# Windowed attention and two expert layers on one core: Q, K and V laid out ahead of the launch, K's key ranges copied from SBUF, score tiles in four banks, early expert products among attention

## The reference, cut to what matters

```python
# q, k, v: [2, 8, 768, 64]; block = 32, window = 16
k_sum = k.reshape(B, H, nb, block, D).max(axis=3)       # 24 block keys
v_sum = v.reshape(B, H, nb, block, D).mean(axis=3)      # 24 block values
scores_l = scale * (q @ k.T) where |i - j| < window, else -1e9
scores_s = scale * (q @ k_sum.T) + log(block)
a = softmax(concat([scores_l, scores_s]))
attn = a @ concat([v, v_sum])
x = attn as [B, S, H*D]                                 # [2, 768, 512]
h = relu(x @ w_in)                                      # w_in [512, 1024]
conv = 3-tap depthwise convolution of h along S
x = (h * sigmoid(conv)) @ w_out                         # w_out [1024, 512]
xn = (x - mean) / sqrt(var + 1e-6) * g_ln
out = x + relu(xn @ w_ch1) @ w_ch2                      # [512, 2048], [2048, 512]
```

## Time and profile before

| | |
|---|---|
| time, median of 3 runs | 463.69 us (462.73 to 463.96) |
| span of the profiled execution, first to last instruction | 460.9 us |
| TensorE busy | 452.0 us, 98% of the span |
| VectorE, ScalarE, GpSimd busy | 275.0, 200.1, 268.3 us |
| first scores on TensorE | 8.37 us |
| last matmul of attention | 80.2 us |
| DMA | 35.28 MB, 57632 of 74725 packets under 512 bytes |

### The profile page before, as it was taken

The page is one execution under the profiler, slowest core; times in us unless marked ns, Lnnn a source line. Parts: engine busy times, 40 slices in busy tenths (PEclk is TensorE's granted clock), DMA queues, the critical chain, the costliest instruction groups (busy, mean ns, idle before and its releaser), DMA issues.

```text
span 460.9 us, 8619 instructions
## 1 busy us (share of the span) xinstructions
PE 452.0 (98%) x3114; PEld 400.5 (87%) x3114; DVE 275.0 (60%) x630; ACT 200.1 (43%) x503; POOL 268.3 (58%) x405
## 2 busy tenths in 40 slices
PE   7899999999999999999999999999999999999997
PEld 6687888989989889989889988998998899889885
DVE  4999976876666967974674254546762244124333
ACT  3898997433335746436243143422421233123210
POOL 2559689999945000097898889750042687878000
PEclk9999999999999999999999999999999999999999
DMA  9998951212102000002115324120020211220003
GB/s 229 213 232 197 195 140 53 92 47 91 47 0 93 0 1 0 1 0 91 54 41 143 109 93 93 67 91 1 26 89 23 93 46 47 91 93 0 1 0 137
DMA packets 74725, 35.28 MB, mean 77 GB/s; under 512 B 57632, under 2 KB 68924, under 8 KB 74684
## 3 DMA queue, kind: packets, MB, share of 16 engines
q1 hardware_dynamic: 71164, 33.85, 27.1%
q10 hardware_dynamic: 3520, 0.88, 0.9%
HBM read 28.83 MB, written 3.15 MB: 69 GB/s over the span
## 4 chain that ended last, share of the span: by engine, by line
PE 96%; DMA 1%; DVE 1%; issue 1%; ACT 1%; ACTq 0%; DVEq 0%
PE two L1689 10%; PE two L1687 10%; PE two L1688 10%; PE two L1664 9%; PE two L1667 8%; PE two L1666 8%; PE two L1460 5%; PE two L1462 5%; PE two L1461 5%; PE two L1595 5%; PE two L1596 5%; PE two L1594 5%; PE two L1413 3%; PE two L1445 3%; PE two L1424 3%; PE two L1342 3%
## 5 line engine op out<-in xcount | busy, mean ns | idle before, releaser
L640 POOL TENSOR_TENSOR asum<-wst 128x256 f32<-128x256 f32 x26 | 21.8, 838 | 93.4 <-PE two L1462 50.2
L1664 PE MATMUL two<-combo,wa 128*128 128x384 f32 x224 | 75.8, 338 | 0.0
L1667 PE MATMUL two<-combo,wa 128*128 128x384 f32 x224 | 75.6, 337 | 0.0
L1666 PE MATMUL two<-combo,wa 128*128 128x384 f32 x224 | 75.2, 336 | 0.0
L1689 PE MATMUL two<-wv,h 128*128 128x512 f32 x192 | 75.0, 391 | 0.0
L1687 PE MATMUL two<-wv,h 128*128 128x512 f32 x192 | 74.8, 390 | 0.2 <-DVE h L946 0.2
L1688 PE MATMUL two<-wv,h 128*128 128x512 f32 x192 | 75.0, 390 | 0.0
L1023 DVE TENSOR_TENSOR u<-two,u 128x384 f32<-128x384 f32 x16 | 8.9, 558 | 90.2 <-PE two L1667 90.2
L1267 ACT ACTIVATE h<-u 128x384 fp32r<-128x384 f32 x16 | 8.4, 525 | 122.4 <-DVE u L1023 122.4
L574 POOL TENSOR_SCALAR pn<-ex,rinv 128x120 f32<-128x120 f32 x96 | 34.8, 383 | 19.1 <-DVE rinv L736 18.4
L634 POOL TENSOR_TENSOR wa<-asum,wa 128x256 fp32r<-128x256 f32 x52 | 43.2, 831 | 4.3
(11 more groups left out here) (119 smaller groups left out, 981.0 us busy)
## 6 DMA issues: line engine op xcount, KB each, us to landing
wst<-in_moe_w_ch SPq DMA_DIRECT2D x26, 512.0 KB, 3.2
vW<-in_v SPq DMA_DIRECT2D x13, 288.0 KB
kn<-in_k SPq DMA_DIRECT2D x15, 192.0 KB, 3.8
qn<-in_q SPq DMA_DIRECT2D x15, 192.0 KB, 3.7
out<-y SPq DMA_DIRECT2D x11, 256.0 KB, 2.0
wst<-in_moe_w_in SPq DMA_DIRECT2D x8, 256.0 KB, 3.1
wst<-in_moe_w_out SPq DMA_DIRECT2D x8, 256.0 KB, 2.8
tok<-xq SPq DMA_DIRECT2D x32, 48.0 KB, 2.0
```

The source lines that it names most:

```text
L1664: nc.tensor.matmul(o, wk[:, 0, kk], ck[:, 0, kk], start=(first and kk == 0), stop=False, skip_group_check=True)
L1666: nc.tensor.matmul(o, wk[:, 0, kk], ck[:, 1, kk], start=False, stop=False, skip_group_check=True)
L1667: ins = nc.tensor.matmul(o, wk[:, 1, kk], ck[:, 0, kk], start=False, stop=(kk == 1), skip_group_check=True)
```

## The change

1. **Layout ahead of the launch.** `kernel()` hands over Q and K already transposed (a pair's 128 dimensions by 768 tokens, K padded by 16 zeros on each side), V with its overlapping windows gathered (96 rows of 6144 bytes a pair), and the two small vectors as columns. `keys_t`, `queries_t`, `queries`, the transpose of the vectors and their PSUM copies are gone. Q lands directly in one of three `qT` tiles (it was two), K in one of two tiles `kT`, one DMA each; V comes by one DMA a pair.
2. **K's ranges from SBUF.** `key_max` and `window_keys` read `kT` in SBUF instead of PSUM, and `window_keys` is one copy of 12 x 96 columns instead of three. For pair 0, ScalarE copies the ranges in three pieces.
3. **Scores in four banks.** The two banks that held transposed K or Q take the scores of odd groups up to group 11, so `scores(n)` waits for the maxima of group n - 2 there, not n - 1.
4. **Order.** The lists of all engines are rewritten down to s = 5. `hidden(0)` begins behind `scores(16)` (it was behind `scores(20)`); `hidden(1)`, `hidden(2)`, half of `hidden(3)` and one tile of `project(0)` stand ahead of the last outputs. The splits of weights on GpSimd begin earlier: 12 of the 32 stand ahead of the last `normalise`, where it was 8.
5. **Fillers.** `fill(i)` is three transposes of the identity, like `warm`: two stand ahead of the first scores and 14 among the first nine groups.
6. `exps` waits for each of a group's four maxima by itself.

```diff
@@ TensorE, helpers @@
-            def transposes(src, dst, done):
-                for t in range(T):
-                    ins = nc.tensor.transpose(dst[:, TOK0 + P * t:TOK0 + P * (t + 1)],
-                                              src[:, t].rearrange("p h d -> p (h d)"), ident[:])
-                ins.then_inc(done, 1)
+            def fill(i):
+                c = P * (i % 4)
+                for k in range(3):
+                    nc.tensor.transpose(ps_o[2][:, c:c + P], ident[:], ident[:])
@@ TensorE, scores @@
-                if n >= 1:
-                    pe.wait_ge(mx_done, GB * n)
+                if n >= 2:
+                    pe.wait_ge(mx_done, GB * (n - 1 if n <= LATE else n))
@@ VectorE @@
-                for b0, nb, w0, nw in ((1, NQ - 2, 0, KEYS), (0, 1, WIN, KEYS - WIN), (NQ - 1, 1, 0, KEYS - WIN)):
-                    nc.vector.tensor_copy(kW[p % 2][:, b0:b0 + nb, w0:w0 + nw], kq_windows(b0, nb, w0, nw)).then_inc(kw_done, 1)
+                nc.vector.tensor_copy(kW[p % 2][:, :, 0:KEYS], k_windows(p, 0, NQ)).then_inc(kw_done, 1)
@@ ScalarE @@
-                act.wait_ge(mx_done, GB * (n + 1))
                 for j in range(GB):
+                    act.wait_ge(mx_done, GB * n + j + 1)
                     ins = nc.scalar.activation(ex[:, n % 2, j], sm[:, n % 2, j], ACT.Exp, bias=mx[:, n % 2, j:j + 1],
@@ SyncE @@
-                for h in range(2):
-                    sp.dma_start(kn[:, p % 2, :, h],
-                                 k[b, 2 * hp + h].rearrange("(t p) d -> p t d", p=P)).then_inc(kn_in[p % 2], 16)
+                sp.dma_start(kT[p % 2][:], k[p]).then_inc(k_in[p % 2], 16)
...
+                sp.dma_start(vW[p % 3][0:KEYS].rearrange("p n d -> p (n d)"), v[p]).then_inc(v_in[p % 3], 16)
@@ kernel() @@
+        if name in ("q", "k"):
+            a = a.transpose(0, 1, 3, 2).reshape(b * h // 2, 2 * d, s)
...
+        if name == "k":
+            a = _np.pad(a, ((0, 0), (0, 0), (win, win)))
+        elif name == "v":
+            a = _np.pad(a, ((0, 0), (win, win), (0, 0)))
+            rows = _np.arange(qb + 2 * win)[:, None] + qb * _np.arange(s // qb)
+            a = a[:, rows].reshape(len(a), qb + 2 * win, -1)
```

More of the change, by code:

```diff
@@ new lines, in _ @@
+            fill(10)
+            block_means(1)
+            fill(11)
+            outputs(0)
+            fill(12)
+            fill(13)
+            scores(5)
+            probs_t(2)
+            outputs(1)
+            probs_t(3)
+            scores(6)
+            scores(7)
+            fill(14)
+            fill(15)
+            outputs(2)
+            probs_t(4)
+            scores(8)
+            block_means(2)
+            probs_t(5)
+            outputs(3)
+            scores(9)
+            outputs(4)
@@ new lines, in _ @@
+            outputs(11)
+            block_means(5)
+            scores(16)
+            probs_t(13)
+            hidden(0, [0, 1, 2, 3])
+            scores(17)
+            outputs(12)
+            outputs(13)
+            probs_t(14)
+            hidden(0, [4])
+            scores(18)
+            probs_t(15)
+            hidden(0, [5])
+            block_means(6)
+            scores(19)
+            probs_t(16)
+            hidden(0, [6])
+            outputs(14)
+            outputs(15)
+            scores(20)
@@ new lines, in _ @@
+            hidden(0, [7])
+            probs_t(17)
+            hidden(1, [0, 1, 2])
+            scores(21)
+            probs_t(18)
+            outputs(16)
+            outputs(17)
+            scores(22)
+            block_means(7)
+            probs_t(19)
+            hidden(1, [3, 4, 5])
+            scores(23)
+            probs_t(20)
+            hidden(1, [6, 7])
+            outputs(18)
+            outputs(19)
+            hidden(2, [0, 1, 2, 3, 4])
+            probs_t(21)
+            hidden(2, [5])
@@ new lines, in _ @@
+            outputs(20)
+            outputs(21)
+            probs_t(22)
+            hidden(2, [6, 7])
+            probs_t(23)
+            project(0, [0])
+            hidden(3, [0, 1, 2, 3])
+            outputs(22)
+            outputs(23)
+            project(0, [1])
+            project(0, [2])
+            project(0, [3])
+            hidden(3, [4, 5, 6, 7])
+            project(0, [4])
+            project(0, [5])
+            project(1, [0])
+            hidden(4, [0, 1])
+            project(1, [1])
@@ L1600, in tokens_t @@
+            hidden(5, [5])
+            project(3, [3])
+            project(3, [4])
+            hidden(5, [6, 7])
+            project(3, [5])
             def tokens_t(slot, dst):
@@ L1612, in tokens_t @@
                 ins.then_inc(xt_ready, 1)
[L1614 removed]
+            for s in range(LISTED, 2 * KF):
                 if s == KF:
```

742 lines of the change are left out of this document (360 added, 382 removed).

## The result

The changed kernel takes 458.52 us in the median of 13 runs (455.96 to 463.50); the kernel before, on the same chips in between, 463.75 us (462.73 to 467.02). The ratio is 0.9892, with a 95% interval of 0.9868 to 0.9916: some 1.1% faster, 5.2 us. The prediction was 455.4 us, so the gain is 5 us where 8 were forecast. All ratios leave out executions more than 1.5% longer than the fastest of the same kernel: here the one of 463.50 us, two of e1 (465.29 and 465.51), one of e5 (1406) and two of e8 (887 and 1812).

A forecast was written before the change was run, and what follows sets the result against it. TensorE was taken as the bound, sharing the pace with VectorE and ScalarE up to scores(16). 42.2 us to there plus 410.4 behind made a 452.6 us span, 8.3 less, so 463.7 - 8.3 = 455.4 us; range 454.2 to 457.2.

The forecast's parts named there:

- the milestone at 42.2 us: Start of scores(16), behind which the expert layer comes in: forecast at 42.2 us, bounds 41.2 and 44.5; 48.40 before.
- TensorE's own sum: TensorE's packed work up to the start of scores(16): 35.7 us from first scores at 6.0, taken as 41.2.
- The allowance: Up to scores(16): 1 us added to 41.2 for engines waiting on each other, where 3.2 were lost before.
- VectorE's 39.5: VectorE's time needed up to scores(16), put near 39 to 40 us, level with ScalarE's 38.5.
- Its own signs: Would be wrong: scores(16) past 45 us, project or hidden waiting for weights, normalise near 1 us, clock under 1.00 before 45.
- rival B: In attention: seven SBUF key copies hold up normalise, 0.6 us each, 4.2 in all; gain 4.1, time 459.6; chance 0.18.
- The first scores: Start of attention on TensorE: first scores near 6.0 us, with K and Q landed in 4 to 5 us.
- Behind the milestone: From scores(16) to the end: 412.5 us less removed and moved blocks leaves 409.4, with allowances 410.4.
- The two allowances: Behind scores(16): 0.5 us for hidden cut into more pieces, 0.5 for small waits for split weights.
- VectorE and the copy of keys: On VectorE: one SBUF copy for three of 1.41 us saves 0.4 each, 1.6 us ahead of scores(16).
- Rival C: First scores to scores(16): TensorE falls to 1.2 GHz while waiting; slower beyond 8.3 of 30 us, 470 at half; chance 0.07.
- The offset: Around the instructions: the median of the runs lies 2.8 us above the span, untouched by the change.

The follow-up runs named there:

- e1: Changed kernel with V of pair 0 loaded ahead of Q of pair 1, K of pair 3 behind the sums of pair 0; 461.60 us, ratio 0.9971 to before.
- e5: Changed kernel with blocks needing no V put ahead of the first two that do, on TensorE, VectorE and ScalarE; 463.04 us, ratio 0.9999 to before.
- e8: Changed kernel with all scores in two banks again instead of four; 461.53 us, ratio 0.9957 to before.
- e3: Changed kernel without V's loads for pairs 3 to 7, which reuse V of pairs 0 to 2; 457.54 us, ratio 0.9868 to before.
- e7: Kernel before with only V gathered into rows of 6144 bytes, one DMA a pair (two for pair 0); ratio 1.0026 to before.
- e9: Changed kernel with the first two loads of expert weights, and GpSimd's first two splits, later; 459.06 us, ratio 0.9907 to before.
- e2: Changed kernel with V of pair 4 loaded ahead of Q of pair 6; 459.19 us, ratio 0.9902 to before.
- e11: e5 with V of pair 2 right behind the sums of pair 0 and V of pair 4 ahead of Q of pair 6; 459.77 us, ratio 0.9913 to before.

## Why the prediction was right in sign and 3 us short

*The step that failed: the milestone at 42.2 us*, and in it the sentence that the three engines TensorE, ScalarE and VectorE set the pace, with 1 us for all waits. The loads were left out: a landing time was taken for the first K and Q alone and none for V, though the earlier trace rows showed a DMA share of 0.96 at 209 GB/s. The change leaves the DMA engines the same 35 MB (35.43 for 35.28) in half as many packets. To 48.4 us they moved 238 GB/s for 216, at a share of 0.84 for 1.00, so some 30% more for each busy microsecond (238 / 0.84 = 283 for 216). They were full from 5 to 20 us; later, at V of pair 4 and in e5 at V of pair 2, TensorE waited for a load that was issued late. Compute lighter by 6 us can't start ahead of its data. The lateness of the profiled milestone, 48.49 - 42.2 = 6.3 us, comes apart like this: first scores 0.5; waits for V and its sums 2.2 + 1.4 = 3.6; waits for ScalarE's copies 1.4; the lower clock about 1.5, from six fillers, scores, outputs and transposed probabilities behind 18 us against the same blocks elsewhere (0.7 + 0.4 + 0.3 + 0.1); less the 1.0 that was allowed for waits. Sum 6.0, and one more gap of 0.3 us stands at 42.59, for which the trace names no releaser. The same account for e3, whose clock was 1.00: 0.3 + 3.1 + 1.1 - 1.0 = 3.5, and 45.79 - 42.2 = 3.6.

*TensorE's own sum held.* Those two accounts close to 0.1 us, so the 41.2 us of packed work was right; it was never reached.

*The allowance was worked out wrongly too.* The 1 us for waits rested on 3.2 us lost before. But the parts that the prediction names for ScalarE (18.2 + 4.7 + 1.3, four copies of Q 2.7, one copy 0.5, one high part 0.3) make 27.7 us and not 29.3; with them 43.6 and not 45.2, and 4.8 us were lost before. For VectorE's 39.5 it shows no sum.

*Its own signs.* Two of the signs of being wrong that it named came true, the milestone past 45 us and a granted clock under 1.00 in the first 45 us; no wait for `wout` or `win` and no mostly slow `normalise` came. The gain of 5.2 us is under its forecast of 6.5 to 9.5 and lies in the band that it gave to rival B, though B isn't what took the 3 us.

*The first scores* came at 6.52 for 6.0, and they waited 1.0 us for ScalarE's ranges of K, which in turn waited for a piece of K of pair 0:

```profile
5.76 0.51 ACT L1070 COPY kW<-kT 128x384 f32<-128x384 f32 x1 [1.39 <-DMA kT<-in_k]
```

Later on K and Q in pieces of twice the size took 6.1 and 5.0 us in the median where the earlier trace rows had 3.8. For V the prediction took no landing time at all; it was 8.0 and 6.4 us for the two loads that TensorE waited for.

*Behind the milestone* 409.4 us were counted and 408.9 measured. The two allowances, 0.5 for more pieces and 0.5 for waits for split weights, weren't needed: two waits of 0.2 us each. That no piece of `project` or `hidden` would wait for its weights was right.

*VectorE and the copy of keys.* Seven copies of 729, 798 and 885 ns (least, median, most), where three copies took 1.41 us: it saves 0.6 each instead of the 0.4 taken.

```profile
L732 DVE COPY kW<-kT x7: 729/798/885, 10.1 to 56.1; 128x1152 f32<-128x1152 f32 x7
```

*Rival B: the hold-up was real, its price wasn't paid.* The 96 `normalise` took 34.8 us before and 38.0 after, with nearly the same median (368 and 364 ns). Before and after, with total and mean:

```profile
L574 POOL TENSOR_SCALAR pn<-ex,rinv 128x120 f32<-128x120 f32 x96 | 34.8, 383 | 19.1 <-DVE rinv L736 18.4 <-PE two L1424 0.6
L568 POOL TENSOR_SCALAR pn<-ex,rinv 128x120 f32<-128x120 f32 x96 | 38.0, 414 | 12.3 <-DVE rinv L763 12.3
```

Before, two of them took over 450 ns, after it nine. Five of the nine start within 0.2 us behind the start of a copy of keys and take 0.78 to 0.94 us. One of these, of 0.94 us, is in this set of four, which would take 1.5 us undisturbed:

```profile
15.71 1.96 POOL L568 TENSOR_SCALAR pn<-ex,rinv 128x120 f32<-128x120 f32 x4 [1.05 <-DVE rinv L763]
16.37 0.81 DVE L732 COPY kW<-kT 128x1152 f32<-128x1152 f32 x1
```

The Trainium skill, SBUF — State Buffer, section Who interferes with whom, says that a VectorE copy in a 2-port mode and a GpSimd instruction exclude each other for the whole instruction. The 0.94 us beside a copy of 0.81 agree. But four of the five stand ahead of the milestone with 1.9 us together over the median, and there TensorE waits for no `normalise`, nor has the chain of waits from 7 to 50 us one in it. So B isn't where the 3 us went, and that the time landed in its band is chance. The prediction's own evidence was misread: the `normalise` of 1075 ns wasn't held up by the cast, which starts first at 78.7 us, behind the last `normalise` at 74.0.

*Rival C was real, in part.* The clock of the kernel before was 1.00 in nearly all of its executions. Of the changed kernel's 13, six were at 1.000, with 457.8 us in the mean; three at 0.996, with 458.7; four below that, with 461.5 to 463.5. In the profiled execution its place is where the prediction put it, behind a wait between the first scores and the milestone, and the fillers there didn't prevent it; it cost 1.5 us. Against the 457.8 us at 1.000 the others are 0.9 us longer at 0.996 and 3.7 to 5.7 below that, but how much of it is the clock and how much the waits that come with it isn't shown. It was priced as all or nothing, at 8.3 us to decide; as a loss of 1 to 6 us in half of the executions it belonged into the forecast.

*The offset.* 2.8 us were put down to what lies around the instructions. Only 1.75 do, in every execution; 1.0 is that the profiled execution of before was the fastest of its three. For the changed kernel the difference is 1.1 us (458.52 - 457.4). So in spans the forecast is 4.8 us short, 457.4 for 452.6, and in medians 3.1; the smaller miss is luck of which executions were profiled.

*What brought the gain.* The four banks are worth about 3 us (e8). Packed V by itself is a loss in the old list (e7). Behind the milestone 3.5 us went, of which 0.8 is the block means that were moved ahead of it; the transposes and their like gave the other 2.7, for 2.3 in the prediction's count. With two banks the worked-out milestone of e8 is 461.53 - 410.75 = 50.8, if its back part is as long, against 49.5 of before. The moved block means explain 0.8 of these 1.3 and the rest is within the noise, so without the four banks 1.5 us less work a pair on TensorE brought nothing there that these runs can tell from noise.

*What stays open.* Removing most of V's bytes (e3), later weights (e9) and an earlier V (e2) each moved the median by 1 us or less, and none of the intervals is apart from the changed kernel's. Shown is that the order on SyncE can cost 3.3 us (e5 against e11) and that the profiled milestone's loss lies in data, the waits that follow from it, and clock. Not shown is what makes executions of the same list differ by up to 7.5 us, what the stop in e2 without a wait is, nor that an order exists which reaches 42 us. No version tried beats the changed kernel.

## What to carry to other kernels

When compute is taken out of a stretch, ask for each load when it is issued and when it lands, and give the forecast a term for it. A DMA share of 0.96 is a reason to look, not an answer: to 48.4 us the share was 1.00 before and 0.84 after, and taking five of V's eight loads away moved the median by 1 us. Read SyncE's list as a list of its own: every load behind a wait is issued no earlier than that wait ends, and moving a block on TensorE, or the copy of its result on VectorE, moves the loads behind it. Where executions scatter by more than the effect, compare medians and not the one profile; a constant part of the program lets each run's time stand in for its profile.

## What the runs showed of the hardware that wasn't expected

- The mean granted clock can lie a little below 1.00 (0.985 to 0.996) in one execution and at 1.00 in the next of the same program. It fell behind waits of 1.4 to 5.0 us: to 0.86 and 0.80 for 5 us each behind 1.4 us, to 0.71 and 0.61 with and behind 5.0 us. It stayed at 1.00 behind waits of 2.3 us in e1 and 1.7 in e11, so the length of one wait doesn't decide it. The kernel before, with no wait over 0.5 us between the first scores and the milestone, stayed at 1.00. The Trainium skill, TensorE: Matmul & The Clock Gate, section HAM oscillation, describes this for longer waits; here it happens in part of the executions only.
- A DMA of 96 rows of 6144 bytes, 576 KB, took 8.0 us behind seven others, 6.4 issued 0.4 us behind Q of one pair, and 9.3 behind 1.7 MB (Q of two pairs, K of one, two halves of weights).
- Little but the sizes of V's rows changed between the kernel before and e7, and the longer rows lost, 464.31 us to 463.44; K's and Q's loads, which didn't change, took 5.6 and 4.9 us for 3.8 and 3.7.
- A `normalise` of 0.36 us that meets a VectorE copy from SBUF of 0.8 us takes 0.78 to 0.94: five of the seven copies held one up.
